# Decayed attention scores on six levels of pairs in place of three levels of fours, ahead of a two-layer expert network

## What is computed

```python
for t in range(S):
    state = alpha[:, :, t, :, None] * state + np.einsum('bhd,bhe->bhde', k[:, :, t], v[:, :, t])
    y[:, :, t] = np.einsum('bhd,bhde->bhe', q[:, :, t], state)
...
for e in range(E):
    h = np.maximum(x @ w1[e], 0.0)
    out += p[:, e:e + 1] * (h @ w2[e])
...
g = h - np.tanh(h)          # h = x @ w_in
return g @ w_out
```

## Time and profile before

| | |
|---|---|
| median of 3 runs | 1383.19 us (1381.79 to 1383.29) |
| profiled execution, time | 1381.91 us |
| its span, first to last instruction | 1380.1 us |
| busy: TensorE, weight loads | 1338.2, 1121.9 us |
| busy: VectorE, ScalarE, GpSimd | 874.3, 573.4, 277.2 us |
| TensorE busy in 0 to 67 us | 33.28 us, mean granted clock 0.77 |
| in 67 to 79.1 us | 8.54 of 12.10 us, clock 1.00 |
| in 79.1 to 1380.1 us | 1296.4 of 1301.0 us, clock 1.00 |
| line 575 (scores), union of its matmuls in units of the main part | 62.7 us |

### The profile page before, as it was taken

How to read it: one execution, slowest core, us unless ns; L and a number is a source line. 1 busy time by engine, 2 the same in 40 slices (tenths; PEclk the granted TensorE clock), 3 DMA queues, 4 the chain that set the end, 5 groups by cost and what they waited for, 6 DMA issues and landing times.

```text
span 1380.1 us, 25841 instructions
## 1 busy us (share of the span) xinstructions
PE 1338.2 (97%) x10177; PEld 1121.9 (81%) x10177; DVE 874.3 (63%) x1767; ACT 573.4 (42%) x1072; POOL 277.2 (20%) x274
## 2 busy tenths in 40 slices
PE   3699999999999999999999999999999999999999
PEld 3578788988878888878898887888887889888888
DVE  8984855994654875465687565497556378323285
ACT  1525346843214751414662323374231476211175
POOL 4666654004022001313001403100221000000000
PEclk8799999999999999999999999999999999999999
DMA  7389797856655656565655655664665465655552
GB/s 217 92 306 321 240 323 242 322 212 219 211 196 197 231 181 218 181 211 196 242 183 179 222 194 199 207 229 169 216 211 172 161 220 189 222 185 200 180 193 89
DMA packets 104680, 289.08 MB, mean 209 GB/s; under 512 B 9936, under 2 KB 64432, under 8 KB 104560
## 3 DMA queue, kind: packets, MB, share of 16 engines
q1 hardware_dynamic: 104416, 287.23, 60.9%
q10 hardware_dynamic: 144, 0.20, 0.1%
HBM read 242.52 MB, written 42.52 MB: 207 GB/s over the span
## 4 chain that ended last, share of the span: by engine, by line
PE 89%; DVE 7%; ACT 2%; issue 1%; DMA 0%; DVEq 0%
PE bank L662 14%; PE bank L663 13%; PE bank L664 13%; PE bank L687 9%; PE bank L688 9%; PE bank L689 9%; PE bank L713 4%; PE bank L711 4%; PE bank L712 4%; PE bank L575 4%; PE bank L616 2%; PE bank L553 1%; DVE RG L1166 1%; PE bank L588 1%; DVE GG L1136 1%
## 5 line engine op out<-in xcount | busy, mean ns | idle before, releaser
L887 ACT ACTIVATE HH<-GG 128x512 fp32r<-128x512 f32 x192 | 121.2, 631 | 631.4 <-PE bank L689 509.2
L662 PE MATMUL bank<-XB,RG 128*128 128x512 f32 x864 | 348.5, 403 | 4.7 <-DVE GG L1109 2.2
L663 PE MATMUL bank<-XB,RG 128*128 128x512 f32 x864 | 339.4, 393 | 0.0
L664 PE MATMUL bank<-XB,RG 128*128 128x512 f32 x864 | 338.3, 392 | 0.0
L1109 DVE SCALAR_TENSOR_TENSOR GG<-bank,PB 128x512 f32<-128x512 f32 x192 | 133.4, 695 | 310.3 <-PE bank L664 310.0
L687 PE MATMUL bank<-HH,RG 128*128 128x512 f32 x576 | 224.3, 389 | 0.0
L688 PE MATMUL bank<-HH,RG 128*128 128x512 f32 x576 | 224.2, 389 | 0.0
L689 PE MATMUL bank<-HL,RG 128*128 128x512 f32 x576 | 224.0, 389 | 0.0
L1320 POOL TENSOR_TENSOR KU<-KU,TOT 128x256 f32<-128x256 f32 x88 | 68.5, 805 | 699.3 <-PE bank L575 699.3
L662 PEld LDWEIGHTS bank<-XB,RG 128*128 128x128 f32 x864 | 162.1, 188 | 45.9 <-issue 4.2
L664 PEld LDWEIGHTS bank<-XB,RG 128*128 128x128 f32 x864 | 162.2, 188 | 35.4
(11 more groups left out here) (129 smaller groups left out, 1676.8 us busy)
## 6 DMA issues: line engine op xcount, KB each, us to landing
RG<-scratch SPq DMA_DIRECT2D x240, 768.0 KB, 4.3
scratch<-RG SPq DMA_DIRECT2D x48, 768.0 KB, 5.3
VS<-vp SPq DMA_DIRECT2D x11, 768.0 KB, 6.0
WS<-w SPq DMA_DIRECT2D x32, 192.0 KB, 3.4
PB<-probs SPq DMA_DIRECT2D x6, 1024.0 KB, 7.0
AU<-qka SPq DMA_DIRECT2D x11, 512.0 KB, 5.3
R<-qka SPq DMA_DIRECT2D x11, 512.0 KB, 5.2
KU<-qka SPq DMA_DIRECT2D x11, 512.0 KB, 6.2
```

The lines of the kernel that those rows point to most:

```text
L662: nc.tensor.matmul(out, w1(g, 0, kt), x_part(m, 0, kt), start=(kt == order[0]), stop=False)
L663: nc.tensor.matmul(out, w1(g, 0, kt), x_part(m, 1, kt), start=False, stop=False)
L664: last = nc.tensor.matmul(out, w1(g, 1, kt), x_part(m, 0, kt), start=False, stop=(kt == order[-1]))
L887: nc.scalar.activation(HH[:, h_slot(g)], GG[:, h_slot(g)], ACT.Copy).then_inc(high, 1)
```

## The change

LEVELS becomes [1, 2, 4, 8, 16, 32]. On each level two sub-blocks join: the second one's queries and the first one's keys take part, so a chunk's 64 keys meet 32 query columns (SW). Queries are kept in one tile (QS, three buffers), and `rotate` is one product in place on every second sub-block; `raise_keys` is one product in place on the others. `tabulate` is one product a level (the total of two neighbours), `distant` is gone, `pick` is two masked copies a level. The key of the first level is raw, and its queries are q times alpha. In the slots a level has one step: SCORES_AT is [1, 2, 4, 5, 7, 8], and at each of these steps TensorE has a burst, VectorE a rotation and a pick, and GpSimd a raise of keys. The burst of a level waits for rotation and keys of the level below.

```diff
-LEVELS = [1, 4, 16]
+LEVELS = [1, 2, 4, 8, 16, 32]
+SCORES_AT = [1, 2, 4, 5, 7, 8]
-SW = CH // 4 * (ROWS - 1)
+SW = CH // 2
...
-            def scores(u, level, half):
...
-                for m in range(UC):
-                    for n in range(2):
-                        c = (2 * half + n) * UC + m
-                        for o, keys, q in crossed(u, c, n):
-                            last = nc.tensor.matmul(fill_bank(u, k + n)[o, m * SW:m * SW + SW], keys,
-                                                    rows[q, c * groups:c * groups + groups, h:ROWS * h],
-                                                    start=True, stop=True)
+            def scores(u, level):
+                if level == 0:
+                    pe.wait_ge(spread[own(u)], turn_of(u) + 1)
+                else:
+                    pe.wait_ge(keys_up[own(u)], NL * turn_of(u) + level)
+                    pe.wait_ge(rotated[own(u)], NL * turn_of(u) + level)
+                bank_free(u, 2 + 2 * level)
+                bank_free(u, 3 + 2 * level)
+                _, second = halves(queries(u)[:, :], LEVELS[level])
+                n = SW // LEVELS[level]
+                for m in range(2 * UC):
+                    for k in range(2):
+                        c = (m // UC * 2 + k) * UC + m % UC
+                        for o, keys, q in crossed(u, c, k):
+                            last = nc.tensor.matmul(fill_bank(u, 2 + 2 * level + k)[o, m * SW:m * SW + SW], keys,
+                                                    second[q, c * n:c * n + n, :], start=True, stop=True)
...
+            def rotate(u, level):
+                first, _, _ = tables(u, level)
+                dve.wait_ge(filled[own(u)], filled_at(u, 3 + 2 * level))
...
+                _, q = halves(queries(u)[:, :], LEVELS[level])
+                nc.vector.tensor_tensor(q, q, first.to_broadcast([P, SPAN[level] // 2, LEVELS[level]]),
+                                        ALU.mult).then_inc(rotated[own(u)], 1)
...
+                if step in SCORES_AT:
+                    rotate(u, SCORES_AT.index(step))
+                    pick(u, SCORES_AT.index(step))
...
 (GpSimd)
-                if step in (3, 6, 9):
-                    raise_keys(u, step // 3 - 1)
+                if step in SCORES_AT:
+                    raise_keys(u, SCORES_AT.index(step))
...
 (ScalarE, prologue)
             lay(0, 0)
             lay(0, 1)
-            join(0)
             lay(1, 0)
             lay(1, 1)
             swap_totals(1)
             act.wait_ge(prob_turned, 1)
             nc.scalar.activation(PT[0:E * NTB * TT, :], bank[3][0:E * NTB * TT, 0:P], ACT.Copy).then_inc(prob_laid, 1)
+            join(0)
             carry_own(0)
```

More of the change, by code:

```diff
@@ L62, with mask_at @@
 REST = C0 - C1 * C1 / (4 * C2)
-def mask_at(level, what):
-    return len(LEVELS) * 96 if what < 0 else level * 96 + (0, 48, 80)[what - 1]
+def mask_at(level):
+    return level * SW
 def level_masks():
@@ L266, in program, with halves, queries @@
         block = ctx.enter_context(nc.Block())
[L268 to L276, removed]
-        def tables(u, level):
[L279 to L283, removed]
+        def halves(ap, h):
+            pairs = ap.rearrange("p (n two h) -> p n two h", two=2, h=h)
+            return pairs[:, :, 0, :], pairs[:, :, 1, :]
+        def queries(u):
+            return QS[2 if own(u) else turn_of(u) % 2]
+        def tables(u, level):
+            t = total(u, level).rearrange("p (n two) -> p n two", two=2)
+            return t[:, :, 0:1], t[:, :, 1:2], total(u, level + 1).rearrange("p (n a) -> p n a", a=1)
         def total(u, level):
@@ L289, in total @@
                 return T64[u % 2][:, :]
[L290 to L302, removed]
+            at = sum(SPAN[1:level])
+            return TOT[own(u)][:, at:at + SPAN[level]]
         def fill_bank(u, k):
@@ L614, in attend @@
                     for hh in range(2):
[L615 removed]
+                        moving = queries(u)[:, c * CH:c * CH + CH] if hh == 0 else QB[own(u)][:, c * CH:c * CH + CH]
                         last = nc.tensor.matmul(fill_bank(u, 18 + n)[CH * hh:CH * hh + D, m * CH:m * CH + CH],
@@ L1274, in _, with tabulate @@
         def _(pool):
-            def tabulate(u, first=0, last=9):
-                n = 9 * turn_of(u)
-                for i in range(first, last):
-                    t, two, three = tables(u, i // 3)
-                    if i:
-                        pool.wait_ge(tabled[own(u)], n + i)
-                    if i % 3 == 0:
-                        out, a, b = two, t[:, :, 0:3], t[:, :, 1:4]
-                    elif i % 3 == 1:
-                        out, a, b = three, two[:, :, 0:2], t[:, :, 2:4]
-                    else:
-                        out, a, b = total(u, i // 3 + 1).rearrange("p (n a) -> p n a", a=1), three[:, :, 0:1], t[:, :, 3:4]
-                    nc.gpsimd.tensor_tensor(out, a, b, ALU.mult).then_inc(tabled[own(u)], 1)
+            def tabulate(u, first=0, last=NL):
+                n = NL * turn_of(u)
+                for level in range(first, last):
+                    one, two, both = tables(u, level)
+                    if level:
+                        pool.wait_ge(tabled[own(u)], n + level)
+                    nc.gpsimd.tensor_tensor(both, one, two, ALU.mult).then_inc(tabled[own(u)], 1)
             def spread_queries(u):
```

304 lines of the change are left out of this document (96 added, 208 removed).

## The result

The changed kernel takes 1392.69 us (median of 4 executions, 1391.39 to 1394.57), the kernel before 1382.49 in the same session (1380.24 to 1383.29): a ratio of 1.0077, 95% interval 1.006 to 1.0095. The profiled execution has a span of 1391.0 us, before 1380.1: **+10.9 us**.

The account below looks back on a forecast made before the run. Behind the prologue TensorE, busy 97% of the span, was taken to bound the kernel. The terms 15.7 - 6.6 + 4.5 - 0.8 = +12.8 us gave a forecast of 1395 us, range 1386 to 1401 with a little over 0.8.

Parts of the forecast that it names:

- The bursts: TensorE's score bursts beside dense work: loading 64 key columns sets the pace, +0.27 us a burst, 58 bursts, +15.7 us.
- the diagonal as a stand-in: TensorE's 32-column burst was priced like the diagonal burst with 64 moving columns, 1.30 us against 1.03 for 96 columns.
- The prologue: Units 0 and 1, computed with nothing beside them, end sooner: -6.6 us, range -8.5 to -3.
- ScalarE then has join(0): Prologue: after the probabilities' transpose and copy, ScalarE runs join(0) 3.7, carries 3.1, join(1) 3.7, to 53.5 against 60.56.
- VectorE's part: Prologue: five rounds at 4.2 us, the last pick 0.9 and the probabilities 2.5 end at 42.4 us.
- the 64 us that the prediction named as a sign of being wrong: End of the prologue: a first expert product later than 64 us would show the prediction wrong.
- The first slots: Slot 2's burst waits for GpSimd's keys of unit 2: +3.5 us, clock 1 (0 to 2), together +4.5 (2 to 6).
- The wait of 0.8: TensorE's longest wait behind the prologue, for masked copies behind step 0's long rotation, goes with that rotation: -0.8 us.
- (a): Rival, TensorE's bursts: the width of the moving data sets the pace; -19 us, 1364, faster; chance 0.12.
- (b): Rival, dense slots: hand-off from level to level is late, fifty times half a microsecond, +25 us, 1420; chance 0.03.
- (c): Rival, TensorE's records: each has a least interval, about 25 ns, 1.6 us a burst; about +54, 1436; chance 0.02.
- (d): Rival: prologue gives more, slot 2 doesn't stall, load at its lower bound; about 0, 1383 us; chance 0.04.

Follow-up runs that it names:

- e1: Changed kernel with 16 of the 32 moving query columns in each burst, half of the scores missing: 1391.32 us, ratio 1.0072 to before.
- e2: Kernel before with 64 of its 96 moving query columns, 32 records a burst as before, some scores missing: 1367.42 us, ratio 0.9901.
- e3: Kernel before with 32 of its 96 moving query columns, 32 records a burst as before, some scores missing: 1366.69 us, ratio 0.989.
- e4: Changed kernel with 32 of the 64 key columns as weights, same count of records, half of the scores missing: 1370.18 us, ratio 0.9925.
- e13: The kernel of e7 profiled a second time, same program: 1391.08 us, ratio 1.0073 to before.
- e7: Changed kernel with GpSimd's low half of weight 7 moved behind the first raise of unit 2's keys: 1392.43 us, ratio 1.0077 to before.
- e10: Changed kernel with e7's edit, and VectorE's first hidden_low moved behind the rotation and picks of slot 1: 1389.39 us, ratio 1.0064 to before.
- e8: Changed kernel with TensorE's turn of unit 0 moved ahead of unit 1's last score burst: 1396.09 us, ratio 1.011 to before.
- e6: Changed kernel, full computation, each level loading only the keys its mask can pick (63 to 32 columns): 1386.48 us, ratio 1.004 to before.
- e9: Changed kernel with the edits of e6, e7 and e8 together: 1385.17 us over 12 executions, ratio 1.002 to before.
- e11: Changed kernel with e10's two edits and e6's trim of the keys: 1381.01 us over 12 executions, ratio 0.9999 to before.
- e12: The changed kernel itself, unaltered, profiled once more: 1391.43 us, one execution.

## Why the prediction was right, point by point

**The bursts: mechanism right, size a little high.** The prediction took the loads of 64 key columns, two in a corner at a time, as the pace, against the width of the moving data. e1, e2/e3 and e4 all say so. +0.27 a burst was predicted; the two ends of D measure 0.22. For 58 bursts that is +12.8, not +15.7. Most of the difference is the diagonal as a stand-in: by one and the same count it costs 1.30 and the 32-column burst 1.26, +0.23. The rest, 0.01, is within what a reading of single bursts can be off. The runs show a load some 58 ns long for 64 columns (64 records start over 1.14 - 0.22 = 0.92 us, in 16 groups of four corners); with 32 columns a group takes some 36 (0.76 - 0.20), and whether that is the load alone isn't shown. The Trainium skill's rule for a load ("TensorE: Matmul & The Clock Gate", "LDWEIGHTS (loading the stationary operand)"), an estimated 53 ns for 64 columns and 27 for 32, has the direction right and is 5 ns short for 64.

**The prologue: the step that failed is ScalarE's start.** -6.6 was predicted, -3.9 measured. The step "ScalarE then has join(0)" had ScalarE free behind the probabilities and their copy, at 43.0. It wasn't: it still had two lays, which wait for TensorE's turns, which wait for the last keys. join(0) started at 45.96, 3.0 later. Behind it all was as predicted: join(0), the carries and join(1) at 10.5 us, measured 10.51 (56.47 - 45.96). In the order before, join(0) started at 46.48, between the lays, and the second lay was done at 52.96. One could have read it from the two orders: with join(0) moved behind both lays, what leads to the lays leads to everything.

VectorE's part was right within half a microsecond (42.4 against 42.86), and that was in part luck: its last masked copies ended at 41.51 and not at 39.9, but the probabilities then took 1.35 us and not the 2.5 of the trace of before.

How much of the 2.7 us between -6.6 and -3.9 belongs to the order can't be said to the tenth, since executions of this same prologue gave 60.38 to 64.77 (five profiles: 63.07, 61.91, 64.77, 60.38, 62.55, mean 62.5, so -4.4 against the one profile before). The range of -8.5 to -3 held four of the five; e13's gave just the -6.6, and e7's came later than the 64 us that the prediction named as a sign of being wrong.

**The first slots.** +4.5 predicted, +3.0 measured by the start of slot 4's burst. The stall came where it was predicted, behind GpSimd's keys, but these were ready at 75.41, +12.3 from the first product, and not at +14.5: ScalarE's high half of weight 7 began at 70.76, +7.7, and not at +9.8. It was half of the story, since VectorE's copies ended 0.1 us ahead of the keys; e7 and e10 show that both must move. By the product behind the stall burst (76.60, +13.5, before +12.1) the keys cost 1.4 and not 3.5. The clock did fall behind the stall: 0.55 in 76.6 to 80.2 us, seven products 0.43 apart instead of 0.23. Against e7, where it stayed up, the stretch to unit 4's diagonal is 1.5 longer; predicted were 0 to 2. Not foreseen was that the first expert products would run at the half clock too: 0.50 in 64 to 66 us, where the kernel before had 1.00 from its first product on. The chain that leads to the late keys runs through them.

**The wait of 0.8** went, as predicted, and no late hand-off took its place.

The sum with measured terms: 12.8 - 3.9 + 3.0 - 0.8 = +11.1, the span says +10.9. The errors of the two large terms had opposite signs (-2.9 and +2.7), so that only the first slots' -1.5 was left: that the total came so near is in part luck.

**The rivals.** (a) fell with e1. (b) had no case. (c) fell with the burst of 1.07 and with e4; its sum in the prediction doesn't come out either, since 1.6 us and the same 0.21 for entry and exit give 58 x 0.78 = +45 for the bursts and +42 in all, not +54. (d) had the prologue at -8 and no stall; neither came.

What stays open: TensorE's gaps in the middle of unit 1's bursts in the prologue, 1.1 us in one profile (after) and 3.9 in another (e7), for which the trace names no releaser. The second lay starts latest in the profile with 3.9, but earliest in e13, which has 1.5, so they are not all of its spread.

## What to carry to other kernels

In these bursts of small matmuls the longer of two times set the pace, streaming the moving columns (96 of them) or loading the weight columns (64, with 64 moving or fewer). Splitting such work into more and narrower pieces pays only until the loads are longer, and then each further record costs its load, so load only the weight columns that the result uses. Where a step is moved in a hand-written order, list what now stands ahead of it, and what leads to that. Where a wait is to be taken away, look at the end times of every engine that feeds the same instruction: two that end within 0.1 us of each other need two moves. To measure a small change in a long kernel, compare stretches between marks of equal work: here such a stretch repeats within 0.1 us from profile to profile, while the whole time scatters by 5.

## What the runs showed of the hardware

- The time of a burst that the weight loads pace follows the clock and the columns. At the granted clock of 0.50 a burst of the prologue took 1.96 us with 64 key columns (profile after) and 1.08 with 32 (e4's timeline, below); beside dense work at 1.00, 1.14 and 0.76.

```profile
30.40 1.08 PE L554 MATMUL bank<-QS,KU 64*32 64x32 f32 x64
```

- TensorE ran its prologue bursts of scores from 17 us on at half speed, though it was busy in 22.83 of the 25 us from 15 to 40 (clock 0.52). In the profiles of e8, e10 and e13 the granted clock reads 1.00 there, yet a record is as long as in the profile after (291 ns against 219 beside dense work), and e6's reads 1.00 over bursts as slow. So the granted clock of a stretch is worth a look at the length or spacing of equal records; here are after's records of the prologue, and then e10's.

```profile
L553 PE MATMUL bank<-QS,KU x320: 282/291/309, 17.1 to 36.2; 64*64 64x32 f32 x160
```

```profile
L553 PE MATMUL bank<-QS,KU x320: 291/291/292, 16.4 to 36.7; 64*64 64x32 f32 x160
```

- The first expert products, which follow a wait of 1.8 to 3.2 us for a DMA, ran at half speed for no time (before, e9) up to 6 us (e8, e11). Behind the stall, products 0.43 us apart instead of 0.23 were seen in all six profiles where TensorE had waited 2.7 to 3.3 us for the stall burst (after, e12, e8, e6, e1, e4), in one of the two with 2.5 (e13, not e7), and in none with 1.8 or less (e9, e10, e11); the kernel before waited 2.2 us at 75.08 and kept its clock. These falls and the start of the second lay go with the scatter ahead of unit 4; behind it there is none.
- VectorE's products of 128x512 took 1.99 and 2.33 us beside GpSimd's (profile after, 69.8 to 74 us), 0.68 and 0.69 at other times.
